# Layer 1 of three mixture experts by seven block products in place of eight, in five of six passes

## The reference, cut to what matters

```python
def _moe_ref(x, domain_probs, w1, w2):      # x (1536, 512), w1 (4, 512, 1024), w2 (4, 1024, 512)
    p = domain_probs / (domain_probs.sum(-1, keepdims=True) + 1e-09)
    out = np.zeros((N, D), dtype=np.float32)
    for e in range(E):
        h = np.maximum(x @ w1[e], 0.0)      # layer 1
        out += p[:, e:e + 1] * (h @ w2[e])  # layer 2
    return out
```

## Time and profile before

| what | value |
|---|---|
| device time, three runs | 754.15 us median, 752.99 to 754.86 |
| span of the profiled execution, first to last instruction | 750.1 us; the page gives no other time of that execution |
| TensorE matmuls / weight loads | 728.0 us (97%) / 606.1 us (81%) busy |
| VectorE / ScalarE / GpSimd | 296.7 (40%) / 209.4 (28%) / 67.0 us (9%) busy |
| mean granted TensorE clock | 0.995 of full |
| read from and written to device memory | 71.0 and 8.2 MB, 106 GB/s on average |

### The profile page before, as it was taken

One profiled execution on the slowest core, in us unless ns is written; L12 is line 12 of the kernel. 1 busy time (PEld: TensorE's weight loads), 2 busy tenths in 40 slices (PEclk: granted clock), 3 DMA queues, 4 the chain that ended last, 5 costly groups with the idle time before them and its releaser, 6 DMA issues.

```text
span 750.1 us, 12660 instructions
## 1 busy us (share of the span) xinstructions
PE 728.0 (97%) x4650; PEld 606.1 (81%) x4651; DVE 296.7 (40%) x874; ACT 209.4 (28%) x504; POOL 67.0 (9%) x97
## 2 busy tenths in 40 slices
PE   5799999999999999999999999999999999999997
PEld 4588898888998989899898989989898986444454
DVE  4878665452432212143221214331514154544341
ACT  4754454451321101032110203222020211543330
POOL 2611000000000000000000000000101002423321
PEclk9999999999999999999999999999999999999999
DMA  9893722213221000022100002252020259599900
GB/s 205 212 218 80 162 56 53 51 28 111 94 77 57 1 0 0 0 81 79 65 0 0 0 0 64 82 192 85 0 85 1 85 207 379 189 402 394 395 29 21
DMA packets 78613, 79.44 MB, mean 106 GB/s; under 512 B 54216, under 2 KB 54492, under 8 KB 78176
## 3 DMA queue, kind: packets, MB, share of 16 engines
q1 hardware_dynamic: 75904, 74.11, 32.0%
q0 software_dynamic: 2656, 4.66, 2.0%
HBM read 71.02 MB, written 8.24 MB: 106 GB/s over the span
## 4 chain that ended last, share of the span: by engine, by line
PE 89%; DVE 5%; DMA 2%; issue 2%; ACT 1%; SPq 1%; DVEq 0%; POOL 0%; POOLq 0%; ACTq 0%
PE ps L1372 23%; PE ps L1374 23%; PE ps L1373 23%; PE ps L1650 6%; PE ps L1678 5%; PE ps L1434 1%; PE ps L1406 1%; PE ps L1568 1%; PE ps L1420 1%; DMA v_first<-stage 1%; PE ps L1385 1%; PE ps L1663 1%; DVE acc L939 1%; PE ps L1557 1%; PE ps L1632 1%
## 5 line engine op out<-in xcount | busy, mean ns | idle before, releaser
L1372 PE MATMUL ps<-xt_hi,w_hi 128*128 128x384 f32 (+1 forms) x508 | 172.9, 340 | 0.0
L1374 PE MATMUL ps<-xt_hi,w_lo 128*128 128x384 f32 (+1 forms) x508 | 170.1, 335 | 0.0
L1373 PE MATMUL ps<-xt_lo,w_hi 128*128 128x384 f32 (+1 forms) x508 | 170.0, 335 | 0.0
L752 ACT ACTIVATE h_hi<-ps 128x384 fp32r<-128x384 f32 x128 | 63.0, 492 | 362.7 <-PE ps L1374 362.6
L1372 PE MATMUL ps<-w_hi,h_hi 128*128 128x512 f32 x384 | 151.9, 395 | 0.0
L1374 PE MATMUL ps<-w_hi,h_lo 128*128 128x512 f32 x384 | 149.9, 390 | 0.0
L1373 PE MATMUL ps<-w_lo,h_hi 128*128 128x512 f32 x384 | 149.8, 390 | 0.0
L985 DVE SCALAR_TENSOR_TENSOR h_lo<-ps,h_hi 128x384 fp32r<-128x384 f32 x128 | 71.2, 556 | 162.2 <-ACT h_hi L752 162.1
L1372 PEld LDWEIGHTS ps<-xt_hi,w_hi 128*128 128x128 f32 x508 | 95.4, 188 | 1.7 <-issue 0.8
L1373 PEld LDWEIGHTS ps<-xt_lo,w_hi 128*128 128x128 f32 x508 | 95.5, 188 | 0.5
L1374 PEld LDWEIGHTS ps<-xt_hi,w_lo 128*128 128x128 f32 x508 | 95.4, 188 | 0.0
(11 more groups left out here) (198 smaller groups left out, 603.4 us busy)
## 6 DMA issues: line engine op xcount, KB each, us to landing
sets<-in_moe_w SPq DMA_DIRECT2D x72, 512.0 KB, 5.2
stage<-in_moe_w SPq DMA_DIRECT2D x24, 512.0 KB, 4.0
stage<-in_k SPq DMA_DIRECT2D x16, 192.0 KB, 4.8
acc<-in_v SPq DMA_DIRECT2D x4, 768.0 KB, 6.5
x_rows<-acc SPq DMA_DIRECT2D x4, 768.0 KB, 3.6
out_rows<-acc SPq DMA_DIRECT2D x4, 768.0 KB, 5.3
acc<-in_moe_w POOLq DMA_DIRECT2D x4, 512.0 KB, 5.6
acc<-in_moe_w SPq DMA_DIRECT2D x4, 512.0 KB, 6.8
```

The costliest lines, as they stand in the source:

```text
L752: nc.scalar.activation(h_hi[:, f, :], ps[:, f % 2, 0:GT], ACT.Relu).then_inc(h_hi_ok, 1)
L1372: mm(dst, a_hi, b_hi, start=start, stop=False)
L1373: mm(dst, a_hi, b_lo, start=False, stop=False)
L1374: return mm(dst, a_lo, b_hi, start=False, stop=stop)
```

## The change

A batch of 768 tokens is now one pass. Its input (512 inner by 768 tokens) is cut into 2x2 blocks, and so is `w1[e]` (512 by 1024). Layer 1 is then made by Winograd's form of the 2x2 block algorithm: seven products of blocks for eight, with sums of weight blocks (S1 to S4), sums of input blocks (T1 to T4) and additions of products. There are six passes (2 batches by experts 1 to 3); the first five use it, and the sixth (batch 1, that is groups 2 and 3, with expert 3) keeps the old form. The order is now by batch first: batch 0 through experts 1, 2, 3, then batch 1 through 1, 2, 3. The hardware loops are gone. In code, `b` of a pass is 0 or 1.

In a pass, `factors` runs four stripes of 128 hidden columns in each half. A stripe is seven products of 6 matmuls of 128x384 each. ScalarE copies four of the PSUM results to SBUF (`put`), VectorE adds PSUM to them (`join`), ScalarE applies the ReLU from SBUF (`high_h`), VectorE makes the low part (`low_hb`). Then `rows_out` makes six tiles of layer 2. The weights of layer 2 are staged in the half of `acc` that belongs to the other batch; batch 1's half is written to device memory first and read back before pass 3 (`SWITCH`). The T sums take the place of batch 1's input in `xt_hi` and `xt_lo`, which is likewise saved (`x_aside`) and brought back. The T3 sums are made on GpSimd (`third_sum`). Routing of groups 0 and 1 stands in passes 3 and 4.

```diff
+    PASSES = [(b, e) for b in range(B) for e in range(1, E1)][:-1]
+    SWITCH = E1 - 1
+    BLOCK_ORDER = (A22, A11, S1, A12, S3, S2, S4)
+    T_ORDER = (T1, T2, T4, T3)
+    ROW_ORDER = [h * FP + i for i in range(FP) for h in range(2)]
+    BX, BZ, BY, BV = 0, 1, 6, 7
...
+        def second_parts(t, i, slot):
+            if t == SWITCH:
+                return ((), (), (), (), (), (0,), (1, 2), (3, 4), (5, 6, 7))[2 * i + slot]
+            return (2 * i + slot - 2,) if 1 <= i < FP else (2 * FP - 2, 2 * FP - 1) if i == FP else ()
...
@@ SyncE @@
-            with sp.Fori(1, E1) as e:
-                load_w1(e, w1[bass.ds(e, 1)])
-                load_w2(e, w2[bass.ds(e, 1)])
+            load_blocks(0)
+            sp.wait_ge(o_lo, TASKS)
+            for j, x in enumerate((xt_hi, xt_lo)):
+                sp.dma_start(x_aside[j], x[:, KC:2 * KC, :].bitcast(F32)).then_inc(x_saved, 16)
...
+            sp.wait_ge(acc_ok, 2 + GR * G)
+            sp.dma_start(late, acc[:, TPH:2 * TPH, :]).then_inc(acc_saved, 16)
+            sp.wait_ge(acc_saved, 16)
+            load_second(0)
+            for t in range(1, len(PASSES)):
+                sp.wait_ge(product, BLOCKS * FP * t)
+                load_blocks(t)
+                if t == SWITCH:
+                    for j, x in enumerate((xt_hi, xt_lo)):
+                        sp.dma_start(x[:, 0:KC, :].bitcast(F32), x_aside[j]).then_inc(x_back, 16)
+                sp.wait_ge(rows_done, TPH * t)
+                if t == SWITCH:
+                    sp.dma_start(acc[:, TPH:2 * TPH, :], late).then_inc(acc_back, 16)
+                    for g in range(HALVES):
+                        keep(g)
+                        send_out(g)
+                    sp.wait_ge(x1_kept, 16 * HALVES)
+                    sp.wait_ge(x1_out, 16 * HALVES)
+                    sp.wait_ge(x1_tr, TPH)
+                load_second(t)
...
@@ GpSimd @@
+            def third_sum(b):
+                (b12, b12_lo), (b22, b22_lo) = x_block(0, 1), x_block(1, 1)
+                to = halves(t_sum_at(b, T3))
+                if b:
+                    gp.wait_ge(x_back, 32)
+                else:
+                    gp.wait_ge(x_saved, 32)
+                    gp.wait_ge(l1_done, FC * G)
+                nc.gpsimd.tensor_tensor(to, b22, b12, ALU.subtract).then_inc(t_pool, 1)
+                gp.wait_ge(t_pool, 3 * b + 1)
+                nc.gpsimd.tensor_tensor(to, to, b22_lo, ALU.add).then_inc(t_pool, 1)
+                gp.wait_ge(t_pool, 3 * b + 2)
+                nc.gpsimd.tensor_tensor(to, to, b12_lo, ALU.subtract).then_inc(t_pool, 1)
...
@@ ScalarE @@
+            def factors(t):
+                for i in range(FP):
+                    n = FP * t + i
+                    if i:
+                        high_h(n - 1, 3, FP + i - 1, 1)
+                    put(n, 1, BY, i, 0)
+                    if i:
+                        high_h(n - 1, 4, FP + i - 1, 0)
+                    put(n, 2, BZ, FP + i, 1)
+                    for k in second_parts(t, i, 0):
+                        high_second(t, k)
...
+                    high_h(n, 1, i, 0)
+                    put(n, 4, BV, FP + i, 0)
+                    put(n, 5, BX, i, 1)
+                    for k in second_parts(t, i, 1):
+                        high_second(t, k)
...
+                    high_h(n, 2, i, 1)
...
@@ VectorE @@
+            def first_sum(b):
...
+                follow(TT(to, b12, b11, ALU.subtract))
+                follow(TT(to, to, b12_lo, ALU.add))
+                TT(to, to, b11_lo, ALU.subtract).then_inc(t_sum, 1)
+            def factors(t):
+                for i in range(FP):
+                    n = FP * t + i
+                    join(n, 1, 3, BX, i, 0)
+                    low_hb(n, 1, i, 0)
+                    for k in (*second_parts(t, i, 0), *second_parts(t, i, 1)):
+                        low_second(t, k)
+                    join(n, 2, 6, BZ, i, 1)
+                    join(n, 3, 7, BX, FP + i, 1)
+                    join(n, 4, 7, BX, FP + i, 0)
+                    low_hb(n, 2, i, 1)
+                    low_hb(n, 3, FP + i, 1)
+                    low_hb(n, 4, FP + i, 0)
...
+            c = G - 1
+            for f in range(FC):
+                low_h(c, f)
+                if f == 1:
+                    first_sum(0)
+                if f == 3:
+                    second_sum(0)
+                if f == 4:
+                    fourth_sum(0)
+                if f == 5:
+                    block_sums(0, 0)
+                if f == 6:
+                    block_sums(0, 1)
+            low_blocks(0, range(3))
+            add_rows(c, 0, c, 0, True)
+            low_blocks(0, range(3, BLOCKS))
+            add_rows(c, 0, c, 1, True)
+            low_sums(0)
+            add_rows(c, 0, c, 2, True)
...
+            for t in range(len(PASSES)):
+                factors(t)
+                more = t + 1 < len(PASSES)
+                add_more(t, 0)
+                if more:
+                    block_sums(t + 1, 0)
+                    block_sums(t + 1, 1)
+                if t >= SWITCH:
+                    choose(t - SWITCH)
+                add_more(t, 1)
+                if t + 1 == SWITCH:
+                    first_sum(1)
+                    second_sum(1)
+                elif more:
+                    low_blocks(t + 1, range(3))
+                else:
+                    low_w1(1, lambda j: stage[:, j, :], [0, 1, 2])
+                add_more(t, 2)
+                if t + 1 == SWITCH:
+                    fourth_sum(1)
+                    low_blocks(t + 1, range(3))
+                if t >= SWITCH:
+                    places(t - SWITCH)
...
+                if t + 1 == SWITCH:
+                    low_sums(1)
+                if t >= SWITCH:
+                    early_sum(t - SWITCH)
+                add_more(t, 5)
+            dve.wait_ge(rows_done, TPH * len(PASSES))
+            low_w1(1, lambda j: stage[:, j, :], [3])
...
@@ TensorE @@
+            def factors(t, fill):
+                for i in range(FP):
+                    n = FP * t + i
+                    block(A12, i, x_of(1, 0), BY)
+                    if n:
+                        pe.wait_ge(joined, 4 * n - 2)
+                    block(S1, i, sum_of(T1), BZ)
+                    fill(2 * i)
+                    if n:
+                        pe.wait_ge(joined, 4 * n)
+                    block(A11, i, x_of(0, 0), BX)
+                    if n:
+                        pe.wait_ge(put_by, 4 * n - 1)
+                    block(A22, i, sum_of(T4), BV)
+                    pe.wait_ge(joined, 4 * n + 1)
+                    block(S2, i, sum_of(T2), BX, True)
+                    pe.wait_ge(put_by, 4 * n + 2)
+                    block(S4, i, x_of(1, 1), BZ, True)
+                    fill(2 * i + 1)
+                    pe.wait_ge(put_by, 4 * n + 4)
+                    block(S3, i, sum_of(T3), BX, True)
...
+            pe.wait_ge(acc_ok, 2 + GR * G)
+            for t in range(len(PASSES)):
+                pe.wait_ge(block_ok, BLOCKS * (t + 1))
+                if t in (0, SWITCH):
+                    pe.wait_ge(t_ok, 4 * (PASSES[t][0] + 1))
...
+            pe.wait_ge(rows_added, TPH * len(PASSES))
```

More of the change, by code:

```diff
@@ L1063, in group, with follow @@
                     add_rows(c, e, g, tt, fresh)
[L1065 to L1068, removed]
+            steps_of_sums = [0]
+            def follow(ins):
+                steps_of_sums[0] += 1
+                ins.then_inc(t_step, 1)
+                dve.wait_ge(t_step, steps_of_sums[0])
+            def first_sum(b):
+                (b11, b11_lo), (b12, b12_lo) = x_block(0, 0), x_block(0, 1)
+                to = halves(t_sum_at(b, T1))
+                if b:
+                    dve.wait_ge(x_back, 32)
+                follow(TT(to, b12, b11, ALU.subtract))
+                follow(TT(to, to, b12_lo, ALU.add))
+                TT(to, to, b11_lo, ALU.subtract).then_inc(t_sum, 1)
@@ new lines, in join, with low_hb @@
+            def join(n, at, made, bank, f, half):
+                dve.wait_ge(product, BLOCKS * n + made)
+                dve.wait_ge(put_by, 4 * n + (1, 4, 2, 3)[at - 1])
+                to = h_raw[:, f, half * GT:(half + 1) * GT]
+                TT(to, ps[:, bank, 0:GT], to, ALU.add).then_inc(joined, 1)
+            def low_hb(n, at, f, half):
+                dve.wait_ge(hb_hi_ok, 4 * n + at)
+                cols = (slice(None), f, slice(half * GT, (half + 1) * GT))
+                nc.vector.scalar_tensor_tensor(out=hb_lo[cols], in0=h_raw[cols], scalar=0.0, in1=hb_hi[cols].bitcast(F32),
+                                               op0=ALU.max, op1=ALU.subtract).then_inc(hb_ok, 1)
@@ L1608, in _, with block @@
             pe.wait_ge(s_const, 15)
-            for g in range(G):
+            def block(j, i, moving, bank, onto=False):
+                hi, lo = moving
+                to = ps[:, bank, 0:GT]
+                for c in range(HALF_D):
```

(20 more changed lines are left out.)

319 lines of the change are left out of this document (265 added, 54 removed).

## The result

The changed kernel takes 751.16 us (median of 6 runs, 749.50 to 752.60), the kernel before 754.07 (6 runs). The ratio is 0.9961, with a 95% interval of 0.9947 to 0.9975. So it is 2.9 us faster, a third of the 8.9 that I forecast, though still inside the range that I gave (739.5 to 752.5). The profiled execution has a span of 748.0 us against 750.1.

A forecast was written before the change was run, and what follows sets the result against it. TensorE's own queue was taken as the bound. 20.8 us saved less 11.9 (0.5 + 3.2 + 0.5 + 5.1 + 0.5 + 2.1) left 8.9, so 754.15 became 745.2 us; range 739.5 to 752.5.

The forecast's parts named there:

- What goes: Layer 1 of the five changed passes: 168 matmuls a pass instead of 192, saving 4.16 us a pass, 20.8 us in five.
- Inside a stripe: Layer 1's 20 stripes: TensorE waits or restarts at tight handshakes between products, 0.5 us lost in all.
- The margins of 0.06 and 0.14: Inside a stripe: time in hand, in us, at the handshakes before product 5 (0.06) and product 7 (0.14).
- the third rival: Handshakes before products 5, 6 and 7 of the stripes miss: 14 us instead of 0.5, total 758.7 us; chance 0.10.
- Into pass 0: Between group 3 and pass 0: VectorE's queue and GpSimd's three operations make the pass start 3.2 us late.
- the hold: Before passes 0 and 3: each of GpSimd's three T3 operations makes VectorE wait for shared ports, 0.8 us each.
- My second rival: GpSimd's two-input operations hold VectorE 1.6 us each before passes 0 and 3: 2.4 more at both, 750.0 us; chance 0.19.
- Pass 0's weights: Layer 2's weights for pass 0, loaded after batch 1's rows are saved, arrive late and cost 0.5 us.
- Before pass 3: Between passes 2 and 3: VectorE's T sums, waiting for `x_back`, and weight blocks outlast `rows_out`; with GpSimd's holds, 5.1 us.
- The clock: Before pass 3: TensorE's idle time could lower its clock, up to 2 us more, not included in the sum.
- Pass 3's own: Within pass 3: layer-2 weights are split last, behind stores and transposes, so TensorE asks before they are ready; 0.5 us.
- the old form's 2.1: Start of the sixth pass: it waits for the last addition and the last weight piece's low part, 2.1 us.

## Why the prediction was wrong

- **What goes, 20.8 us: right.** Every undisturbed pass takes 61.90 us.
- **Inside a stripe, 0.5: it was 0.** `join` starts 3.34 us into a stripe (284.77 for the pass of 281.43) where I had 3.32. The margins of 0.06 and 0.14 hold in all stripes of pass 1, so the third rival falls.
- **Into pass 0, 3.2: it was 5.1, and 1.6 of clock behind it. This is the first step that failed.** The term mis-sized is the hold by GpSimd's operation, 0.8 us by the cast of the earlier trace rows: each held VectorE by 1.5, so 4.4 and not 2.4 came into the queue. The mechanism was as the prediction put it, and taking GpSimd's sums out gave back 3.4 us there. My second rival had this, with 1.6 a hold; its 750.0 is the rival's time nearest to the 751.16 measured (750.6 by the estimate of 1.7), but partly by luck, as it had neither the clock nor the late `x_back`. The operation itself lasts 2.6 to 2.7 us there, longer than the hold, so I also should not have taken the one for the other. The Trainium skill's GPSIMD Engine Reference, section "Elementwise — side-by-side cycle accounting", gives an estimate of 1.7 us by its figure for 2048 columns. The trace has 1.85 where GpSimd begins with VectorE idle and 2.4 to 2.7 where the two take turns.
- **Pass 0's weights, 0.5: 0**, since pass 0 itself was late. They are 0.5 late once it isn't.
- **Before pass 3, 5.1: pass 3 starts 9.1 late, 7.6 of waits and 1.5 of slow clock between them. The second failed step.** Of the 4.0 more, 2.1 is the hold again (4.5 and not 2.4), and 1.7 is `x_back`: `first_sum` starts 17.0 us behind the end of the products (389.44 and 372.48) where I had 15.3. VectorE then runs without a pause until pass 3 starts. I also looked only at the pass's start, and not at the tiles: the addition of tile 2 stands behind the T sums, and most of the wait came there. The end of the sums is the same, so this alone doesn't cost more, but it makes one long idle time.
- **The clock, named as up to 2 us at one place and put at nothing in the sum: 1.6 us, at the other place. The third failed step.** It fell at two. Behind the wait into pass 0, where I hadn't named it, the 1.6 us come on top. Before pass 3, where I had, the 1.5 lie in time in which VectorE holds TensorE anyway. The row for it was there, 0.93 granted in the first 50 us; I should have put a price to every wait of 3 us.
- **Pass 3's own 0.5, and the old form's 2.1: 0.5 and 2.3.** Right.

So 11.9 us of costs were 18.6, and 8.9 became 2.1 in spans, 2.9 in medians. The medians' 0.8 beyond the spans needs no cause of its own: single executions differ by 3 us, and one of each kernel was profiled.

## What to carry to other kernels

Where an algorithm saves TensorE's time with work on the vector side, a stripe's balance is the easy part: the loss sits where the queue of the helper has to finish everything at once. There, wait for each operand by itself, let no operation that waits for a transfer stand in front of one that frees a bank, and keep GpSimd's operations that read SBUF away from a vector queue that sets the end: moving three of them a batch onto the loaded engine, as two, gained 5.5 us. And count each idle time of TensorE of some 3 us at its length plus 1.6, unless another engine holds TensorE behind it anyway.

## What the runs showed of the hardware

- A GpSimd operation with two inputs of 128x768 takes 1.85 us where it begins with VectorE idle, and 2.4 to 2.7 when they take turns; each VectorE operation of 768 columns on two SBUF inputs behind it takes 2.5 instead of 0.96 us. VectorE's `low_h`, which reads PSUM and SBUF, kept its 0.55 us between them. A GpSimd fill of the same size (0.74 us) holds nothing.
- Nine TensorE waits of 3.0 to 5.2 us stand in the first mixture of these profiles, and behind all nine the granted clock was at half, for 3.4 us and once (a wait of 5.0) for 6.8; where such a wait was filled with matmuls into an unused bank it stayed full. Behind shorter waits it isn't settled by the length: it fell in three profiles of seven behind the old form's wait (2.1 us, 2.3 with the restart), and behind the transposes' wait of 1.9 us in pass 3 in one of three.
- A slow stretch of 3.4 us costs 1.5 to 1.6 us (1.2 in the one behind the transposes' wait), and nothing when VectorE holds TensorE behind it anyway.
